# An mLSTM and two MLP layers on one core: 82-column products for the even heads of the first two chunks, and two unread products between those chunks' sums

## The reference, cut to what matters

```python
for t in range(S):
    m_new = np.maximum(f_gate[:, :, t] + m, i_gate[:, :, t])
    f_stab = np.exp(f_gate[:, :, t] + m - m_new)
    i_stab = np.exp(i_gate[:, :, t] - m_new)
    C = f_stab * C + i_stab * einsum('bhd,bhe->bhde', vt, kt)
    n = f_stab * n + i_stab * kt
    h_tilde = einsum('bhde,bhe->bhd', C, qt)
    nq = einsum('bhd,bhd->bh', n, qt)
    y[:, :, t] = sigmoid(o_gate) * h_tilde / np.maximum(np.abs(nq), 1.0)
```

## Time and profile before

| | us |
|---|---|
| median of 3 runs | 598.75 |
| lowest and highest of them | 597.57, 599.56 |
| the profiled execution, its own time | 597.8 |
| its span, first to last instruction | 596.1 |
| PE busy, PE weight loads busy | 586.9 (98%), 531.9 (89%) |
| VectorE, ScalarE, GpSimd busy | 237.2, 201.0, 104.1 |
| mean granted TensorE clock | 0.997 |

### The profile page before, as it was taken

The page is one execution under the profiler, slowest core; times in us unless marked ns, Lnnn a source line. Parts: engine busy times, 40 slices in busy tenths (PEclk is TensorE's granted clock), DMA queues, the critical chain, the costliest instruction groups (busy, mean ns, idle before and its releaser), DMA issues.

```text
span 596.1 us, 8943 instructions
## 1 busy us (share of the span) xinstructions
PE 586.9 (98%) x3660; PEld 531.9 (89%) x3660; DVE 237.2 (40%) x474; ACT 201.0 (34%) x396; POOL 104.1 (17%) x75
## 2 busy tenths in 40 slices
PE   8999999999999999999999999999999999999998
PEld 7899999989988888899999999999999999999997
DVE  6566757676655333413132313131323131323222
ACT  5675645555534444611113311113311111111111
POOL 3868201111000244420003400004400000000000
PEclk9999999999999999999999999999999999999999
DMA  6978544554220133210001210001000000001011
GB/s 252 347 241 279 221 111 134 169 158 112 58 50 27 38 98 104 93 58 0 1 1 48 98 49 1 1 1 48 1 0 1 2 0 1 1 0 45 1 44 46
DMA packets 35343, 43.84 MB, mean 74 GB/s; under 512 B 18670, under 2 KB 27878, under 8 KB 35302
## 3 DMA queue, kind: packets, MB, share of 16 engines
q1 hardware_dynamic: 35302, 43.26, 22.6%
HBM read 38.85 MB, written 4.40 MB: 73 GB/s over the span
## 4 chain that ended last, share of the span: by engine, by line
PE 90%; DVE 5%; issue 1%; DMA 1%; SPq 1%; ACT 1%; DVEq 0%
PE bank L1125 10%; PE bank L1126 10%; PE bank L1124 10%; PE bank L1175 9%; PE bank L1176 9%; PE bank L1174 9%; PE bank L1128 5%; PE bank L1127 5%; PE bank L1145 4%; PE bank L1147 3%; PE bank L1146 3%; PE bank L1153 1%; PE bank L1154 1%; PE bank L963 1%; PE bank L974 1%
## 5 line engine op out<-in xcount | busy, mean ns | idle before, releaser
L940 DVE SCALAR_TENSOR_TENSOR g_lo<-bank,g_hi 128x512 fp32r<-128x512 f32 x96 | 66.3, 691 | 254.2 <-ACT g_hi L659 254.2
L659 ACT ACTIVATE g_hi<-bank 128x512 fp32r<-128x512 f32 x96 | 57.5, 599 | 270.5 <-PE bank L1128 270.4
L1175 PE MATMUL bank<-w_all,g_hi 128*128 128x320 f32 x384 | 118.8, 309 | 0.0
L1176 PE MATMUL bank<-w_all,g_lo 128*128 128x320 f32 x384 | 118.6, 309 | 0.0
L1124 PE MATMUL bank<-x_hi,w_all 128*128 128x512 f32 (+2 forms) x318 | 117.2, 369 | 1.3 <-DVE x_hi L841 1.3
L1174 PE MATMUL bank<-w_all,g_hi 128*128 128x320 f32 x384 | 118.5, 309 | 0.0
L1126 PE MATMUL bank<-x_hi,w_all 128*128 128x512 f32 (+2 forms) x318 | 118.4, 372 | 0.0
L1125 PE MATMUL bank<-x_lo,w_all 128*128 128x512 f32 (+2 forms) x318 | 118.3, 372 | 0.0
L480 POOL TENSOR_TENSOR w_all<-w_raw,w_all 128x1408 fp32r<-128x1408 f32 x16 | 51.6, 3227 | 232.6 <-ACT w_all L542 232.6
L1175 PEld LDWEIGHTS bank<-w_all,g_hi 128*128 128x128 f32 x384 | 72.2, 188 | 3.8
L1174 PEld LDWEIGHTS bank<-w_all,g_hi 128*128 128x128 f32 x384 | 72.2, 188 | 3.7
(11 more groups left out here) (134 smaller groups left out, 644.0 us busy)
## 6 DMA issues: line engine op xcount, KB each, us to landing
w_raw<-in_w SPq DMA_DIRECT2D x24, 704.0 KB, 4.1
feat<-in_feat SPq DMA_DIRECT2D x12, 512.0 KB, 4.7
tok<-in_tok SPq DMA_DIRECT2D x12, 484.0 KB, 5.6
zb<-z SPq DMA_DIRECT2D x10, 512.0 KB, 4.5
out<-arena SPq DMA_DIRECT2D x12, 160.0 KB, 1.9
spare<-xg SPq DMA_DIRECT2D x7, 256.0 KB, 2.6
fb<-f SPq DMA_DIRECT2D x14, 80.0 KB
xg<-feat SPq DMA_DIRECT2D x14, 80.0 KB
```

Of the source, the lines that this page charges most:

```text
L659: A(g_hi[:, b, 0:N], h_ps[b][:, 0:N], ACT.Relu).then_inc(ghi_ready, 1)
L940: V.scalar_tensor_tensor(g_lo[:, b, 0:N], h_ps[b][:, 0:N], 0.0, g_hi[:, b, 0:N].bitcast(F32), ALU.max, ALU.subtract).then_inc(g_ready, 1)
L1175: mm(out, g_hi[:, b, t], low_w, start=False, stop=False)
L1176: last = mm(out, g_lo[:, b, t], high_w, start=False, stop=stop)
```

## The change

In `intra`, the product of an even head of chunks 0 and 1 passes by the columns of V of its own head and of the odd head behind it, 82 in place of 41, and writes 82 columns of the bank. The product of the odd head comes later in TensorE's order and starts its 41 columns anew, so what the even head's product wrote there is overwritten. For chunks from 2 on nothing changes. Between `intra(0)` and `intra(1)` stand two `keep_warm` products, into `bank[3]`, without a wait of their own.

```diff
                 for q in range(2):
                     pe.wait_ge(p_done, 2 * n + q + 1)
                     for h in range(q, HEADS, 2):
-                        last = mm(o_ps[:, h * HDE:(h + 1) * HDE],
+                        end = D + (h + (2 if n < BATCH and q == 0 else 1)) * HDE
+                        last = mm(o_ps[:, h * HDE:end - D],
                                   pwork[:, n % 2, q, (h // 2) * CH:(h // 2 + 1) * CH],
-                                  tok[:, r, D + h * HDE:D + (h + 1) * HDE], start=True, stop=True)
+                                  tok[:, r, D + h * HDE:end], start=True, stop=True)
                 last.then_inc(intra_ready, 1)
@@
             intra(0, c_ps)
+            keep_warm(2, bank[3])
             intra(1, up_ps[0])
             turn(0, c_ps)
             weigh_columns()
```

## The result

| | before | after |
|---|---|---|
| median of 16 runs each, us | 598.34 | 597.02 |
| lowest and highest | 597.47, 600.18 | 596.30, 598.57 |
| profiled execution, its own time and span | 597.8, 596.1 | 597.01, 595.3 |
| mean granted clock of that execution | 0.997 | 1.000 |

The ratio is 0.9973 with a 95% interval of 0.9962 to 0.9984: 1.3 us or 0.27% faster, clear of no change, a little inside of the 0.3% of the prediction. The forecast was 598.1 us with a lower end of 597.2; the measured time lies 0.2 us under that end. The direction was right and the size about half of what came.

What follows compares the result with a forecast made beforehand. TensorE, busy 586.9 of 596.1 us, was taken as the bound, with one half-clock stretch to win back. +0.1 - 0.44 - 0.34 = -0.7 us, from the 598.75 us median, gave 598.1 us; range 597.2 to 599.7.

Steps and rivals of the forecast that it cites:

- The sum: Whole kernel: +0.1, -0.44 and -0.34 make -0.7 us, taken from the three-run median 598.75 to give 598.1 us.
- +0.1 us for the two products: Between the sums: the pause hides most of the two 512-column products, `intra(1)` starts about 0.1 us late; bounds 0 and 0.45.
- -0.44 for `intra(1)`: Chunk 1's sums: with the clock held at 1.00 they take 1.95 us instead of 2.39.
- -0.34 for `turn(1)`: Four transposes before `x_high(1)`: 0.59 us at full clock instead of 0.93.
- The 82 columns: Even heads' products in both `intra`: wider products taken as 0 us extra, at most 0.1 us for each chunk.
- ScalarE's L540 and GpSimd's L469 and L477: Work beside the chain that might eat the gain: L540 would end near 17.0 us, L469 and L477 early enough.
- the clock term: From 14.4 to 17.8 us: denser work holds clock 1.00, saving 0.44 us in `intra(1)` and 0.34 in `turn(1)`.
- The third rival: Half clock at a dearer place (the MLP products again) in other runs; gain up to 1.7 us, 597.05 us; chance 0.12.
- The first rival: At 14.4 to 17.8 us the clock falls as before; +0.1, at most +0.5 us, 598.85 us; chance 0.25.
- The second rival: The clock falls later, onto the first MLP products; +0.4 us, 599.15 us, or 599.75 with the ceiling; chance 0.13.

Runs made afterwards that it cites:

- the last chain above: Chain of the changed kernel run once more, with no further edit, beside the wide products alone; 597.07 us, ratio 0.9973 against the kernel before.

## Why the prediction missed: one stretch was read, the median has two

**The sum held, for the execution that it was read from.** The forecast had +0.1 us for the two products, -0.44 for `intra(1)` and -0.34 for `turn(1)`, together -0.7. Measured: +0.08 for the products (10.64 against 10.56), -0.44 for `intra(1)` (2.39 to 1.95 in the wide products alone), and from `turn(1)` to `x_high(1)` 18.14 - 17.18 = 0.96 us before and 17.92 - 17.23 = 0.69 after, -0.27, together -0.63. The four transposes took 17.61 + 0.27 - 17.23 = 0.65 us, not the 0.59 of the later place. The 82 columns cost nothing, as put. ScalarE's L540 and GpSimd's L469 and L477 did not swallow the gain: from `intra(0)` to `x_high(1)` it is 17.18 - 10.51 = 6.67 us in the last chain above against 18.14 - 10.84 = 7.30 before, the same 0.63 us.

**The step that failed** is the clock term, -0.44 - 0.34 us, sized on one stretch of half clock and then carried over in the part "The sum": "It stands 0.95 us under the median of the three runs. I take the same difference from the median". That took the gain of one execution for that of the median, as if both had the same thing to lose. The profiled execution had one half-clock stretch, from 14.4 to 17.8 us. By their mean clock 66 of 111 runs had two (in the execution that I later saw, from 13.2 to 20.0 us), and from such a run there are 12.02 - 10.64 = 1.4 us to take. The median gave 1.3. The 0.95 us by which the profiled run stood under the median fits the second stretch, since the medians by clock, 597.47 and 598.68 us, are 1.2 us apart; no clock is listed for those three runs.

A second thing moved the range: its base, the median of three runs, lay at 598.75 us, and that of the sixteen at 598.34. The measured gain taken from 598.75 would have given 597.4 us, inside the range; that the time fell outside is in part the luck of three runs. The gain itself was twice the forecast either way.

**The rivals.** The third rival named this mechanism, half clock at a dearer place in most runs, with its ceiling of 1.7 us (two stretches in fact cost 1.7 us), and got a chance of 0.12 because one trace showed one stretch. The three times at hand, up to 2 us apart, and a profiled run below the median by more than the forecast gain deserved more. The range ended at 597.2 us, just short of that rival's own 597.05. The first rival (the wider products don't hold the clock) is what happens in 4 of 24 runs with the wide products alone, and in none of 28 with the two added, unless the run that recorded 0.949 is one (its 597.33 us do not look like it). The second rival, the later fall, was not seen in the changed kernel, though it is real without the three products around `turn(1)`.

For that rival I had weighed a rule of the Trainium skill ("TensorE: Matmul & The Clock Gate", Part 4, PE-mode transpose), by which transposes don't bring about the full clock. In the changed kernel the stretch of 14.4 to 17.6 us (the last of the sums, ten transposes, one unread product and a wait) stayed at 1.00, and by their mean clock 27 of 28 runs had no such stretch at half clock; transposes ran at either level, the last of a turn in 0.27 us at 1.00 and in 0.42 us at 0.50. The traces do not agree with a rule that strict, though none isolates what transposes do to the clock. A thing that the same page says would have helped: in Part 1 it holds that the point at which the clock changes is not tied to the kernel's start and differs from run to run. The traces agree: of the same kernel before, the clock fell at 14.4 us in one execution and at 13.2 in another.

**What stays open.** Why some runs of several kernels record 0.991 or 0.989 and take 600 to 603 us: no profile caught one. Why columns that are overwritten hold the clock at all: the runs show that they do, not by what. How the hold divides between the odd heads and the pause. And whether the medians by clock (0.5 us for the first stretch, against 0.7 in the stage) mean that the later waits at 100 to 150 us take up a part of a gain; they swing too much in single profiles to tell.

No variant was shown to beat the changed kernel: all held runs, whatever the edit, have medians of 596.8 to 597.1 us, except where six products were added. What the change buys is that nearly every run is a held one.

## What to carry to other kernels

When a gain hangs on the granted clock, one profile shows one of several outcomes: sort the times of many runs by their mean clock before sizing it, and take the spread of the runs as a sign of what the profile does not show. The narrow float32 products of this kernel are not paced by their columns up to 82, so widening them over columns that are overwritten later held the clock in 20 of 24 runs, against 9 of 111, at no cost; at 164 columns they began to cost. Added products are free only up to the length of the pause that they fill. Read the gain of a small edit from the stage, between two events on the chain, and not from the span, which here swung by over a microsecond for other reasons.

## What the runs showed of the hardware that was not expected

The pace of these float32 products did not depend on width from 41 to 82 columns (1.95 us for 16 whether none or eight of them have 82, mean duration 278 and 276 ns); with 164 it did (2.12 us for 16 of which six have 164, mean 318 ns). At half clock the 41-column products went from 1.95 to 3.47 us for 16, so their pace follows TensorE's clock although at these widths it does not follow their columns.

The share of time for which TensorE is recorded busy does not foretell the fall here: it was 3.11 of 3.40 us ahead of it in the kernel before, 2.95 of 3.40 us at the same place in the changed kernel, which held 1.00.

What half clock costs depends on what it lies on. Falls of two stretches cost 2.3 us from 12.6 us on, with the two added products under it, and 1.7 us from 13.2 us and from 13.9 us on; of single ones, that at 14.4 us cost 0.7, its greater part lying beside VectorE's work, and that at 19.1 us 1.2, on the MLP products.
